# Attention, a routed expert layer and a dense layer on one core: routing moved into the attention batches, sorted rows kept as the dense stage's input, scores computed transposed on halves of the array

## What is computed

```python
# attention: x (8 batches, 8 heads, 512 rows, 64), state (8, 8, 32, 64)
scores = scale * x @ state.T            # softmax over the 32 states
xread  = softmax(scores) @ state        # 512 rows of a batch
scores2 = scale * state @ x.T           # softmax over the 512 rows
sread  = softmax(scores2) @ x           # 32 rows of a batch
x = concat([xread, sread]) as (8 * 544 = 4352 rows, 512)
# expert layer: 8 experts, w1 (8, 512, 1024), w2 (8, 1024, 512)
logits = (x / norm(x)) @ (emb / norm(emb)).T / tau
expert = argmax(logits); gate = softmax(logits)[expert]
out[rows of e] = gate * (relu(x[rows of e] @ w1[e]) @ w2[e])
# dense layer: w_in (512, 2048), w_out (2048, 512)
g = s * relu(x @ w_in) ** 2 + b
return g @ w_out                        # (4352, 512), float32
```

## Time and profile before

| | us |
|---|---|
| median of 3 runs | 1500.07 (1498.54 to 1501.28) |
| span of the profiled execution | 1499.6 |
| TensorE busy in it | 1396.4 (93%) |
| TensorE's mean granted clock | 0.965 of full speed |
| VectorE, ScalarE, GpSimd busy | 534.1, 509.6, 193.3 |

### The profile page before, as it was taken

The page is one execution under the profiler, slowest core; times in us unless marked ns, Lnnn a source line. Parts: engine busy times, 40 slices in busy tenths (PEclk is TensorE's granted clock), DMA queues, the critical chain, the costliest instruction groups (busy, mean ns, idle before and its releaser), DMA issues.

```text
span 1499.6 us, 20856 instructions
## 1 busy us (share of the span) xinstructions
PE 1396.4 (93%) x6774; PEld 1160.5 (77%) x6775; DVE 534.1 (36%) x801; ACT 509.6 (34%) x882; POOL 193.3 (13%) x251
## 2 busy tenths in 40 slices
PE   6999518999999999999499999999999999999998
PEld 5888406888888888887488888888888888888886
DVE  3566681144422144131632232323323232232322
ACT  4677502244433244243232222222222222222221
POOL 1111331222222222221600000000000000000000
PEclk7999758999999999999699999999999999999999
DMA  8677313124432124213101010100101010010000
GB/s 208 177 199 224 103 15 141 42 100 152 148 142 104 42 93 150 98 36 147 47 1 42 1 56 0 56 0 0 56 0 56 0 47 9 0 56 0 29 1 28
DMA packets 88456, 105.22 MB, mean 70 GB/s; under 512 B 44262, under 2 KB 59622, under 8 KB 87921
## 3 DMA queue, kind: packets, MB, share of 16 engines
q1 hardware_dynamic: 82160, 85.52, 18.3%
q0 software_dynamic: 6272, 19.41, 3.8%
HBM read 78.15 MB, written 27.80 MB: 71 GB/s over the span
## 4 chain that ended last, share of the span: by engine, by line
PE 51%; DVE 1%; DVEq 0%; issue 0%; ACT 0%
PE ps_g L1404 25%; PE ps_o L1422 25%; PE ps_yt L1392 1%; DVE w_out_lo L1367 1%; DVE w_raw L1360 0%; DVE g_lo L1350 0%; DVE y_lo L1339 0%; PE ps_o L1440 0%; DVE sq L1347 0%; DVEq L1449 0%; ACT rel L1311 0%; DVEq L1363 0%
## 5 line engine op out<-in xcount | busy, mean ns | idle before, releaser
L1347 DVE TENSOR_TENSOR sq<-rel 128x512 f32<-128x512 f32 (+1 forms) x144 | 97.3, 676 | 492.7 <-ACT rel L1311 492.6
L1311 ACT ACTIVATE rel<-ps_g 128x512 f32<-128x512 f32 (+1 forms) x144 | 82.8, 575 | 534.4 <-PE ps_g L1404 534.4
L1404 PE MATMUL ps_g<-y_hi,w_in_hi 128*128 128x512 f32 (+1 forms) x576 | 218.8, 380 | 3.7 <-DVE y_lo L1339 3.6
L1404 PE MATMUL ps_g<-y_lo,w_in_hi 128*128 128x512 f32 (+1 forms) x576 | 218.2, 379 | 0.0
L1404 PE MATMUL ps_g<-y_hi,w_in_lo 128*128 128x512 f32 (+1 forms) x576 | 218.1, 379 | 0.0
L1422 PE MATMUL ps_o<-w_out_hi,g_hi 128*128 128x512 f32 x544 | 213.4, 392 | 0.6 <-DVE g_lo L1350 0.6
L1422 PE MATMUL ps_o<-w_out_lo,g_hi 128*128 128x512 f32 x544 | 211.9, 389 | 0.0
L1422 PE MATMUL ps_o<-w_out_hi,g_lo 128*128 128x512 f32 x544 | 211.7, 389 | 0.0
L1404 PEld LDWEIGHTS ps_g<-y_hi,w_in_hi 128*128 128x128 f32 x576 | 109.3, 190 | 25.3 <-DVE y_lo L1339 4.0
L1404 PEld LDWEIGHTS ps_g<-y_lo,w_in_hi 128*128 128x128 f32 x576 | 109.3, 190 | 20.6 <-issue 0.2
L1404 PEld LDWEIGHTS ps_g<-y_hi,w_in_lo 128*128 128x128 f32 x576 | 109.3, 190 | 20.0
(11 more groups left out here) (215 smaller groups left out, 1737.7 us busy)
## 6 DMA issues: line engine op xcount, KB each, us to landing
w_raw<-in_moe_w SPq DMA_DIRECT2D x16, 2048.0 KB, 9.7
out_rows<-w_raw SPq DMA_DIRECT2D x34, 256.0 KB, 2.1
x_a<-in_x SPq DMA_DIRECT2D x8, 1024.0 KB, 7.4
x_tok<-x_rows SPq DMA_DIRECT2D x8, 1024.0 KB, 5.5
y_rows<-moe_tok SPq DMA_DIRECT2D x8, 1024.0 KB, 5.6
x_m<-in_x SPq DMA_DIRECT2D x7, 1024.0 KB, 9.5
w_raw<-in_moe_w_out SPq DMA_DIRECT2D x1, 4096.0 KB, 14.9
w_raw<-in_moe_w_in SPq DMA_DIRECT2D x1, 3072.0 KB, 14.3
```

The source lines that it names most:

```text
L1311: nc.scalar.activation(rel[:, k, 0:cols], ps_g[k][:, 0:cols], ACT.Relu).then_inc(rel_ready, 1)
L1347: nc.vector.tensor_tensor(sq[:, 0:cols], rel[:, k, 0:cols], rel[:, k, 0:cols], ALU.mult).then_inc(sq_ready, 1)
L1404: last = nc.tensor.matmul(ps_g[n % 2][:, 0:cols], w[:, wc], a[:, c, 0:cols], start=(c == 0 and w is w_in_hi and a is y_hi), stop=(c == DC ...
```

## The change

There is one block instead of three. The parts:

- **Scores**: TensorE makes the transposed scores first, as products of 64 output partitions with 512 columns, two of which fill the two halves of PSUM's partitions; the row-wise scores come from 8 transposes of them. The reads of states and tokens are also made in halves (`p`). State transposes are made once at the start.
- **Routing per batch**: `choose` and `place` find expert and slot of a batch's 544 rows on VectorE, one and two batches late, in steps that wait for each other; POOL writes the row numbers with five indirect DMAs into `slot_tab`, 4352 slots per expert. A short table of tiles is made at the end. Rows in `x_tok` are 544 floats: 512 values and four partial logits per expert.
- **Experts**: per tile POOL loads the row numbers (`tile_ids`), keeps them (`keep_ids`), gathers into one buffer `xg`, and stores the result in sorted order. Gates are computed per tile (`gate_square`, `gate_scale`, `gate_soft`, `gate_final`) and are applied at the result. TensorE turns tile g+2 before `up` of g+1.
- **Weights**: w1, w2 of expert 0 are split during attention; w_in is loaded and split in 8 pieces, one per expert; w_out in 16 pieces, from the end of the experts into the first dense group.
- **Dense**: takes the sorted rows; the results go out with one indirect DMA per tile by POOL.
- **Places**: `line_pad` rounds the small tensors up to a multiple of 128 bytes; all tensors of the expert and dense products then start at a multiple of 128.

```diff
+        used = sum(-(-n // 32) * 32 for n in (4 * P, 4 * P, 2 * P, 2 * P, 4 * PAIRS * E, 4 * RW, ...))
+        sb(top, "line_pad", [P, (-(-used // 128) * 128 - used) // 4], f32)
...
+            for bb in range(B):                                    # gpsimd
+                pool.wait_ge(pos_ready, bb + 1)
+                for t in range(TPB + 1):
+                    n = P if t < TPB else NS
+                    nc.gpsimd.indirect_dma_start(out=slot_tab[:, :],
+                                                 out_offset=bass.IndirectOffsetOnAxis(ap=pos5[0:n, t:t + 1], axis=0),
+                                                 in_=ids[0:n, bb, t:t + 1], in_offset=None).then_inc(slots_written, 16)
+            def tile_ids(g, first):
+                if not first:
+                    pool.wait_ge(gathered, 16 * g)
+                    pool.wait_ge(id_stored, 16 * g)
+                pool.dma_start(g_idx[:], slot_tab[0:P, :] if first else slot_tab[ds(slots_of(pool, g), P), :])\
+                    .then_inc(idx_loaded, 16)
+                pool.wait_ge(idx_loaded, 16 * g + 16)
+            def next_tile(g):
+                tile_ids(g, False)
+                keep_ids(g)
+                pool.wait_ge(tab_ready, 1)
+                pool.wait_ge(xg_tr, g)
+                pool.wait_ge(gate_sq, g)
+                pool.wait_ge(gate_lg, g)
+                gather(g)
+            with pool.Fori(1, last) as g:
+                next_tile(g + 3)
+                store(g)
...
+            def tile(g):                                           # scalar
+                hidden(g + 1)
+                x_hi(g + 2)
+                next_w1(g + 1)
+                result(g)
+                gate_soft(g + 2)
+                act.wait_ge(gate_ready, g + 3)
+                gate_square(g + 3)
+                hidden_hi(g + 1)
+                next_w2(g)
...
+            def place(bb):                                         # vector, 4 small steps
+                dve.wait_ge(rank_mm, bb + 1)
...
+            def choose(bb):                                        # vector, 12 small steps
+                dve.wait_ge(rows_ready, 2 * TPB * (bb + 1))
...
+            def gate_scale(g):                                     # vector, 17 small steps
+                dve.wait_ge(gathered, 16 * g + 16)
...
+            def tile(g):
+                x_lo(g + 2)
+                next_w1(g + 1)
+                gate_final(g + 2)
+                hidden_lo(g + 1)
+                next_w2(g)
+                gate_scale(g + 3)
...
+            def scores(i):                                         # tensor
+                for jj in range(2):
+                    for par in range(2):
+                        p = slice(HP * par, HP * par + HP)
+                        last = nc.tensor.matmul(bank_t[jj][p, :], st_t[:, i, jj, p], x_t[:, 2 * jj + par, :], start=True, stop=True)
+            def state_read(bb):
+                            last = nc.tensor.matmul(bank_r[p, jj * P:(jj + 1) * P], a2_n[:, t, jj * P + HP * par:jj * P + HP * par + HP],
+                                                    x_m[bb % 3][:, t, j * P:(j + 1) * P], start=(t == 0), stop=(t == TPB - 1))
+            def token_read(bb):
+                            last = nc.tensor.matmul(read_bank[t % 2][par][:, jj * GW:(jj + 1) * GW], a1_t[p, jj, t * P:(t + 1) * P],
+                                                    st_pair[p, bb, jj, :], start=True, stop=True)
+            for i in range(B):
+                scores(i)
+                if i >= 2:
+                    ranks(i - 2)
+                if i >= 1:
+                    state_read(i - 1)
+                state_emb(i)
+                turn_scores(i)
+                if i + 1 < B:
+                    for j in range(PAIRS):
+                        x_transpose(i + 1, j)
+                if i >= 1:
+                    turn_rows(i - 1)
+                turn_e2(i)
+                if i >= 1:
+                    token_read(i - 1)
+                    row_logits(i - 1)
+                turn_a1(i)
...
+            def tile(g):
+                turn_hidden(g)
+                turn_x(g + 2)
+                up(g + 1)
+                down(g)
...
+            down(last_g)
+            dense(0, HEAD, True)
...
+                    nc.gpsimd.indirect_dma_start(out=out[:, :],
+                                                 out_offset=bass.IndirectOffsetOnAxis(ap=out_id[:, r:r + 1], axis=0),
+                                                 in_=o_sb[:, k, :], in_offset=None).then_inc(o_stored, 16)
-        blk.close()
-        blk = ExitStack()
-        block = blk.enter_context(nc.Block())
```

More of the change, by code:

```diff
@@ L940, in attention_moe_ffn @@
[L940 to L957 removed]
+        win_loaded = sem("win_loaded")
@@ new lines, in _ @@
+            sp.wait_ge(win_ready, E)
+            sp.wait_ge(moe_stored, 16 * (HEAD + E + 2))
+            sp.wait_ge(id_stored, 16 * (HEAD + E + 2))
+            load_y(0, HEAD)
+            with nc.allow_non_contiguous_dma(reason="one word per row"):
+                load_ids(0, HEAD)
+            last = last_tile(sp)
+            sp.wait_ge(moe_stored, 16 * last + 16)
+            sp.wait_ge(id_stored, 16 * last + 16)
+            sp.sem_inc(load_turn, 1)
+            sp.wait_ge(gate_sq, last + 3)
@@ new lines, in _ @@
+            AHEAD = 4
+            rows_hi(0, HEAD, False)
+            for n in range(AHEAD):
+                wout_hi(n)
+            result(last)
+            for n in range(FC2):
+                gate_hi(0, n, HEAD * P)
+                if n + AHEAD < FC2:
+                    wout_hi(n + AHEAD)
+            rows_hi(1, TROWS, True)
+            with act.Fori(1, NFULL) as u:
+                for n in range(FC2):
+                    gate_hi(u, n, TROWS * P)
+                rows_hi(u + 1, TROWS, True)
@@ new lines, in state_emb @@
+            def state_emb(i):
+                if i >= 1:
+                    pe.wait_ge(se_ready, i)
+                else:
+                    pe.wait_ge(emb_done, 1)
+                if i >= 2:
+                    pe.wait_ge(pos_ready, i - 1)
+                for jj in range(2):
+                    for par in range(2):
+                        p = slice(HP * par, HP * par + HP)
+                        last = nc.tensor.matmul(bank_l[p, L_SE + jj * E:L_SE + jj * E + E], st_t[:, i, jj, p],
+                                                emb_t[:, 2 * jj + par, :], start=True, stop=True)
+                last.then_inc(se_mm, 1)
@@ new lines, in _, with turn_x @@
+            ranks(B - 2)
+            state_read(B - 1)
+            turn_rows(B - 1)
+            token_read(B - 1)
+            row_logits(B - 1)
+            ranks(B - 1)
+            nc.tensor.matmul(bank_r[:, 0:E], ones_b[:], pre5[:, TPB + 1, :], start=True, stop=True).then_inc(tot_mm, 1)
+            def turn_x(g):
+                pe.wait_ge(gathered, 16 * g + 16)
+                if starts(g):
+                    pe.wait_ge(rows_ready, 2 * TPB * B)
+                else:
+                    pe.wait_ge(xg_ready, g)
+                for c in range(DC):
+                    last = nc.tensor.transpose(ps_xt[:, c * P:(c + 1) * P], xg[:, row_col(c):row_col(c) + P], ident[:])
+                last.then_inc(xg_tr, 1)
```

1803 lines of the change are left out of this document (830 added, 973 removed).

## The result

The changed kernel takes **1672.89 us** (median of 4 runs, 1669.43 to 1677.52), the kernel before 1499.3. The ratio is 1.1154, 95% interval 1.1131 to 1.1177: 11.5% slower, where 1382 and faster had been forecast. The profiled execution has 1676.0 us.

What follows compares the result with a forecast made beforehand. TensorE was taken as busy nearly all the time in four stretches and mostly waiting elsewhere. 1499.6 - 6 (attention) - 36 (routing) - 20 (experts) - 22 (turnover) - 2 (first group) - 33 (dense) + 2 (end) = 1382; range 1350 to 1455.

Steps and rivals of the forecast that it cites:

- The sign: Whole kernel: the change makes it faster, chance 0.95; same 0.01, slower 0.04.
- the expert step: Expert stage: 20 us less, from -33 products, +9 start, +5 expert changes, -1 last tile's turn.
- The cover of the gather: Expert loop: the gather lands near 10 us after `down` ends, is needed at 12.5; 2 us of slack.
- Rival (c): Experts: the one buffer `xg` becomes the bound, which ends slower; 4 us a tile, 1534 us; chance 0.05.
- Padding: Expert and dense products: operands starting at multiples of 128 bytes take 0.216 us each, 33 us less in each stage.
- rival (b): Products: only the 32-byte offset matters; experts reach 0.2267 (13 of 33 us), dense stays; 1438 us; chance 0.13.
- Attention: Attention stage: batches of 17.0 us, last a1 transposes end at 154 instead of 160.2, 6 us less.
- (d): Attention: array halves run side by side and VectorE is quick enough; batch 15.9 instead of 17.0, 1374 us; 0.64 including forecast.
- Routing: Between attention and experts: 33 us in series instead of 69.1, 36 less; first product near 187.
- Turnover: Between experts and dense: barrier, row loading, scaling, transposing and splitting half of w_out go, -22 us.
- first group: First dense group: 49 us instead of 51.4, -2, with POOL's sums slowing VectorE as before.
- end: End of kernel: four results by indirect DMA on POOL's queue, 7.4 us instead of 5.4, +2.

Runs made afterwards that it cites:

- ids_copy: The changed kernel with the store of 128 row numbers ahead of the gather replaced by one 512-byte copy in DRAM from slot_tab to moe_id: 1550.7 us.
- ahead_copy: The changed kernel with a second gather buffer, the row-number list loaded two tiles ahead, and the DRAM copy replacing the small stores: 1485.9 us, ratio 0.9918.

## Why the prediction was wrong

**The sign: the expert step.** The cover of the gather ("Covered, with 2 us of slack; if that cover goes, each us late costs 38 us") failed. The first input of the round was the price of a gather, 3.7 us from the earlier trace rows: here it was 10.1, for the store of four-byte words ahead of it, which I had listed as one more issue on POOL and priced at nothing. A write of that form was among the things the trace of before did not show, and it should have had a bound from above. The second was the index load, whose 2.3 us at the median was right but which stands in the round with its issue, the wait for `gathered` and the store. The third was the order on ScalarE: I had put the square ahead of the high parts as 0.8 us of work, not as a wait that a late gather passes on to `hid_hi`, the splits and the next gather. No run undoes this third alone; the trace shows the wait (4.1 us in the round above). Undone one by one, by the stage's length from first to last product: changed 694.5 us, words replaced by the copy 562.7, list ahead 538.2, second buffer 496.5. So the stores of four-byte words made 132 of the 198 us, and with them gone the cover holds within an expert.

What then remains is a second term: a change of expert was priced at 0.7 us, 5 in all. In ids_copy the 21 tiles at the changes take 324 us, 61 more than at the 12.5 of the others, and even with two buffers (ahead_copy) 23 more.

**Rival (c) was the case**, and I had given it 0.05. It had priced 4 us a tile on top of the forecast; the stage came out at 694.5 us where the forecast has 482.3 - 20 = 462.3, 6.1 a tile more, 0.5 of them the padding that brought less. The slack was stated (2 us) and so was its price (38 us for each us late), while three numbers in the round were guesses. A cover of 2 us on a round of 12.5 does not earn 0.05 for its failure. The "against" in (c), that gathers took 3.7 us beside the same loads, rested on a kernel without such stores.

**Padding** (-33 in the experts, -33 in dense) failed. The lines of 128 bytes and 17/16 fitted the dense figure exactly, and dense did not move: 2.72 per twelve before and after. No ten products of 512 fp32r columns in a row came under 0.2265 each. In the experts there was a gain of 0.007 a product, by the other mechanism (agreement modulo 256). The distances are thus those of rival (b), in size too (13 us), with the wrong reason. A formula that hits a number to the digit was taken as evidence, with one number to fit it to.

**Attention**: the a1 transposes end at 157.1, not 154. The halves run side by side, as (d) had it, but a batch takes (139.11 - 49.37) / 5 = 17.9 us, not 15.9 to 17.0: the shorter list leaves TensorE waiting for ScalarE and VectorE (16.5 us busy of 19.0 from 86 to 105), and it comes back at a lower clock, 0.85 over the stage where the earlier trace rows had 0.93. The stage ended only 3.1 us later than forecast because two errors partly cancel: the start and the first batch took 3.4 us less than counted (second batch at 31.57 instead of 35), the seven others 6.5 more. That is luck.

**Routing** came to 43.7 us instead of 33: the last scatter to `slot_tab` lands 7.8 us after its issue, where 3.7 stood in the sum, and the index load took 6.1 with its issue instead of 2.5. These are 7.7 of the 10.7 us; the other 3 were not traced. Four-byte words go out here too, though no run without them shows that they are the cause (timeline of POOL):

```profile
180.50 0.86 POOL L454 DMA_INDIRECT slot_tab<-ids,pos  x1 [0.30 <-issue]
188.26 0.59 POOL L462 DMA_DIRECT2D g_idx<-slot_tab  x1 [6.90 <-DMA slot_tab<-ids,pos]
194.33 1.02 POOL L467 DMA_INDIRECT xg<-x_tok,g_idx  x1 [5.47 <-DMA g_idx<-slot_tab]
```

**Turnover** was right, -22.1. The **first group** takes 58.5, not 49: POOL's sums (L509) now meet VectorE's split and low parts at once. A low part of 256 columns takes 1.37 us beside them and 0.42 after:

```profile
899.82 21.19 POOL L509 TENSOR_TENSOR b_row<-b_row,w_raw 128x512 f32<-128x512 f32 x14
```

```profile
916.79 1.37 DVE L1034 TENSOR_TENSOR g_lo<-sq,g_hi 128x256 fp32r<-128x256 f32 x1
...
922.72 0.42 DVE L1034 TENSOR_TENSOR g_lo<-sq,g_hi 128x256 fp32r<-128x256 f32 x1
```

The slowing was read correctly before, but spread over the group's 50 us instead of counted where the chunks wait for it. The **end** took 6.6 more instead of 2: four scatters go out 1.27 us apart.

With the expert loop mended (ahead_copy, 1485.9) the forecast would still have been 104 us too low. The larger parts: dense 33 and its first group 9 (both as in the changed kernel), the experts' products 1824 x (0.2273 - 0.216) = 21, the rest of the expert stage about 14, and the first product at 204.5 instead of 187.

## What to carry to other kernels

A store that moves one four-byte word per partition to DRAM cost others more than itself here: look for it ahead of any transfer that someone waits for, and try such a list as a copy from DRAM to DRAM, which did no such harm. Before taking a buffer away, write down the whole round from release to refill, each engine's order included. If its slack is smaller than the doubt in one of its terms, treat the round as the bound. Price the rare tile, here the change of expert, by the same round and not by its own work alone. Where each transfer had a buffer of its own, the engines' time rose 2.4 times and TensorE stood still only in the last tile.

## What the runs showed of the hardware that I had not expected

- Stores of 128 words of four bytes raised the landing of a gather from 3.5 to 10.1 us and that of 2 MB of weights from 9.7 to between 13 and 15, on another queue. The same 512 bytes as runs of 32, from DRAM, left both alone.
- A product of 512 fp32r columns takes 0.2267 to 0.2291 us if its two operands start at the same place modulo 256 bytes, and 0.2338 to 0.2349 where they are 128 or 96 apart (other distances were not tried), at the three common places tried (64, 128, 192).
- Products on the two halves of the array ran side by side (1.94 us for eight records of 512 columns). The Trainium skill (TensorEngine Tiling (Array Packing), Key Properties) has tiles load and multiply independently; this trace agrees.
